# Attention and two mixture-of-experts layers in one kernel: w1 split by quarters, scatters without a wait between halves, and the first expert's weight splits of layer 2 moved

## The reference

```
cur = np.einsum('bhd,bhe->bhde', u[None] * kt, vt)
y[:, :, t] = np.einsum('bhd,bhde->bhe', rt, state + cur)
state = wt[:, :, :, None] * state + np.einsum('bhd,bhe->bhde', kt, vt)
...
h = np.maximum(x[mask] @ w1[e], 0.0)
out[mask] = gate_w[mask, None] * (h @ w2[e])
...
for k in range(2):
    mask = top2[:, k] == e
    h = np.maximum(x[mask] @ w1[e], 0.0)
    out[mask] += top2_w[mask, k, None] * (h @ w2[e])
```

## Time and profile before

| | us |
|---|---|
| median of 3 runs (lowest, highest) | 1000.42 (1000.36, 1000.91) |
| time of the profiled execution | 1001.47 |
| its span in the profile | 999.8 |
| TensorE matmul busy | 910.0 |
| VectorE busy | 540.0 |
| ScalarE busy | 228.8 |
| GpSimd busy | 350.7 |
| mean granted TensorE clock, share of full | 0.958 |

### The profile page before, as it was taken

The page is one execution under the profiler, slowest core; times in us unless marked ns, Lnnn a source line. Parts: engine busy times, 40 slices in busy tenths (PEclk is TensorE's granted clock), DMA queues, the critical chain, the costliest instruction groups (busy, mean ns, idle before and its releaser), DMA issues.

```text
span 999.8 us, 22055 instructions
## 1 busy us (share of the span) xinstructions
PE 910.0 (91%) x7285; PEld 881.0 (88%) x7286; DVE 540.0 (54%) x950; ACT 228.8 (23%) x417; POOL 350.7 (35%) x364
## 2 busy tenths in 40 slices
PE   5999999999999999681499999999999999999994
PEld 5888888899999999571499899998998999999894
DVE  8888998784333343249753444435436354543532
ACT  2232333112110121154121312213113131311210
POOL 7333334324322223103434343433534343343232
PEclk9999998999999999795599999999999999999998
DMA  6676782129111102451263444424424444422232
GB/s 246 203 233 217 267 279 78 54 60 360 49 49 40 55 32 64 123 182 47 52 211 56 106 104 115 100 52 108 110 40 102 118 102 114 106 48 42 39 55 42
DMA packets 54447, 111.46 MB, mean 111 GB/s; under 512 B 8688, under 2 KB 35568, under 8 KB 54384
## 3 DMA queue, kind: packets, MB, share of 16 engines
q1 hardware_dynamic: 34752, 71.07, 21.4%
q0 software_dynamic: 15744, 34.70, 17.2%
q10 hardware_dynamic: 3888, 4.89, 1.3%
HBM read 84.84 MB, written 25.81 MB: 111 GB/s over the span
## 4 chain that ended last, share of the span: by engine, by line
PE 85%; DVE 10%; issue 2%; DMA 2%; ACT 0%; DVEq 0%; POOL 0%; POOLq 0%
PE ps L1640 22%; PE ps L1642 22%; PE ps L1641 22%; PE ps L1550 3%; PE ps L1510 2%; PE ps L1514 2%; PE ps L1479 2%; PE ps L1456 2%; DVE weights L1089 2%; PE ps L1541 2%; PE ps L1504 1%; PE ps L1565 1%; PE ps L1577 1%; DVE grow L893 1%; PE ps L1464 1%
## 5 line engine op out<-in xcount | busy, mean ns | idle before, releaser
L1640 PE MATMUL ps<-x_hi,weights 128*128 128x256 f32 x984 | 280.1, 285 | 12.3 <-DVE x_lo L1361 12.3
L1642 PE MATMUL ps<-x_hi,weights 128*128 128x256 f32 x984 | 279.2, 284 | 0.0
L1641 PE MATMUL ps<-x_lo,weights 128*128 128x256 f32 x984 | 279.1, 284 | 0.0
L822 ACT ACTIVATE hid_hi<-ps 128x512 fp32r<-128x512 f32 x164 | 98.3, 599 | 567.3 <-PE ps L1642 567.3
L1640 PE MATMUL ps<-weights,hid_hi 128*128 (+1 forms) x616 | 214.2, 348 | 1.4 <-DVE hid_lo L1366 1.1
L1366 DVE SCALAR_TENSOR_TENSOR hid_lo<-ps,hid_hi 128x512 fp32r<-128x512 f32 x164 | 112.7, 689 | 184.4 <-ACT hid_hi L822 184.4
L1642 PE MATMUL ps<-weights,hid_lo 128*128 (+1 forms) x616 | 207.3, 337 | 0.0
L1641 PE MATMUL ps<-weights,hid_hi 128*128 (+1 forms) x616 | 207.2, 336 | 0.0
L1640 PEld LDWEIGHTS ps<-x_hi,weights 128*128 128x128 f32 x984 | 188.2, 191 | 14.4 <-DVE x_lo L1361 11.4
L1641 PEld LDWEIGHTS ps<-x_lo,weights 128*128 128x128 f32 x984 | 188.4, 191 | 0.0
L1642 PEld LDWEIGHTS ps<-x_hi,weights 128*128 128x128 f32 x984 | 188.2, 191 | 0.0
(11 more groups left out here) (279 smaller groups left out, 1076.8 us busy)
## 6 DMA issues: line engine op xcount, KB each, us to landing
stage<-in_moe_w_dram SPq DMA_DIRECT2D x18, 1536.0 KB, 7.4
kv_in<-in_kv_T_dram SPq DMA_DIRECT2D x24, 512.0 KB, 5.6
kv_in<-in_kv_T_dram SPq DMA_DIRECT2D x24, 448.0 KB, 3.5
w_in<-in_w_T_dram SPq DMA_DIRECT2D x24, 258.5 KB, 4.2
out_dram<-zeros SPq DMA_DIRECT2D x25, 192.0 KB, 8.5
x_rows<-y_tok ACTq DMA_DIRECT2D x24, 192.0 KB, 4.7
stage<-moe_rows SPq DMA_DIRECT2D x12, 384.0 KB, 5.0
stage<-in_moe_w_dram SPq DMA_DIRECT2D x2, 768.0 KB, 7.7
```

What stands on the lines that cost most here:

```text
L822: act.activation(hid_hi[:, 2 * q:2 * q + 2, :], h_ps[q], ACT.Relu).then_inc(s_hhi[l], 1)
L1640: pe.matmul(out_ps, hi, by_hi, start=first, stop=False)
L1641: pe.matmul(out_ps, hi, by_lo, start=False, stop=False)
L1642: return pe.matmul(out_ps, lo, by_hi, start=False, stop=final)
```

## The change

There are three parts. **w1 by quarters:** at a change, ScalarE copies quarter q of w1 right behind `hidden_high(s, q)` and VectorE subtracts it right behind `hidden_low(s, q)`; TensorE waits for each quarter by itself. The same holds for the first expert of layer 2. In layer 1's first expert the halves stay. The first `split_x` now stands behind the fourth `hidden_low`, and VectorE's lookups behind the first one instead of the second. **Spare rows:** the empty places of the second half of a step name another 128 rows, `out` is 128 rows longer, and the wait between a step's two scatters is gone; the scatters of a step wait for both scatters of the step before. **Start of layer 2:** GpSimd's `split_w2(0)` stands behind the third gather, two quarters of VectorE's `low_w1` ahead of the lists' code and two behind the `split_x`, and `low_w2` behind `slot_tables`.

```diff
-        spare_row = [sb("spare_row0", [P, NTX[0]]), sb("spare_row1", [P, 1])]
+        spare_row = [sb("spare_row0", [P, NTX[0]]), sb("spare_row1", [P, TS])]
...
+        def w1_quarter(tile, at, q):
+            return tile[:, at:at + WSZ].rearrange("p (c f) -> p c f", c=CC)[:, :, q * F // 4:(q + 1) * F // 4]
...
                     load_w2(l, e)
-                    sp.wait_ge(s_w1lo[l], n * 2)
+                    sp.wait_ge(s_w1lo[l], n * 4)
...
-                    for g in range(G + 1):
+                    for g in range(G + TS):
                         clear(g)
...
                 if l == 1:
-                    split_w2(0)
                     pool.wait_ge(s_table[l], 1)
...
                     if l == 1 and not (isinstance(s, int) and s == 0):
-                        pool.wait_ge(s_scatter[l][1 - u][TS - 1], j * 16 + u * 16)
+                        for t in range(TS):
+                            pool.wait_ge(s_scatter[l][1 - u][t], j * 16 + u * 16)
...
                         else:
-                            if t > 0:
-                                pool.wait_ge(s_scatter[l][u][t - 1], j * 16 + 16)
-                                pool.nop(nofuse=True)
                             pool.indirect_dma_start(out=out, out_offset=where, in_=sy[u][:, t, 0:C], in_offset=None,
...
                 if l == 0:
                     first_w2()
                 else:
+                    split_w2(0)
                     pool.wait_ge(s_table[l], 3)
...
+            def split_w1(l, n, q):
+
+                act.wait_ge(s_w1[l], loaded(l, n, 1))
+                act.activation(w1_quarter(weights, W1_HI, q), w1_quarter(w1_raw, 0, q), ACT.Copy).then_inc(s_w1hi[l], 1)
...
-                    for q in range(1, 4):
-                        hidden_high(s, q)
-                    with act.If(change > 0):
-                        act.wait_ge(s_h[l], s * 4 + 4)
-                        act.nop(nofuse=True)
-                        for a in range(2):
-                            split_w1(l, run + 1, a)
+                    for q in range(4):
+                        if q:
+                            hidden_high(s, q)
+                        with act.If(change > 0):
+                            split_w1(l, run + 1, q)
...
-                    low_w1(1, 0, 0)
-                    low_w1(1, 0, 1)
+                    for q in range(2):
+                        low_w1(1, 0, q)
                     dve.wait_ge(s_code[l], 1)
...
                     split_x(0, 0, 0)
                     split_x(0, 0, 1)
+                    for q in range(2, 4):
+                        low_w1(1, 0, q)
+                    slot_tables(1)
                     low_w2(1, 0)
-                    slot_tables(1)
                     loop_ends(1)
...
                     hidden_low(s, 0)
-                    hidden_low(s, 1)
                     if runs_from(l, s):
...
+                        for q in range(4):
+                            if q:
+                                hidden_low(s, q)
+                            if q == 3:
+                                split_x(s + 1, 1 - u, 0)
+                            with dve.If(change > 0):
+                                low_w1(l, run + 1, q)
...
                     if runs_from(l, s):
-                        with dve.If(change > 0):
-                            for a in range(2):
-                                low_w1(l, run + 1, a)
                         split_x(s + 1, 1 - u, 1)
...
                 def up(s, q, run):
 
-                    pe.wait_ge(s_w1lo[l], run * 2 + 2)
+                    pe.wait_ge(s_w1lo[l], 4 if l == 0 and isinstance(s, int) and s == 0 else run * 4 + q + 1)
                     pe.wait_ge(s_sxc[l], s * TS + TS)
```

More of the change, by code:

```diff
@@ L685, in _ @@
                     pool.wait_ge(s_mixst, 16)
-                    pool.wait_ge(s_zero, 16 * (G + 1))
+                    pool.wait_ge(s_zero, 16 * (G + TS))
                     gather(0, 0, 0)
@@ L746, in attention_step @@
                 if late(b, c) in (6, 7):
-                    split_w1(0, 0, late(b, c) - 6)
+                    first_w1(late(b, c) - 6)
                 if late(b, c) in (8, 9):
@@ L1339, in _ @@
                        .then_inc(s_table[l], 1)
-                    link(dve.tensor_scalar(idx_tmp[:, 0:NSl], empty[:, 0:NSl], spare_row[l][:, 0:1], None, ALU.mult))
+                    link(dve.tensor_tensor(idx_tmp[:, 0:NSl].rearrange("p (s t) -> p s t", t=TS),
+                                           empty[:, 0:NSl].rearrange("p (s t) -> p s t", t=TS),
+                                           spare_row[l][:, :].unsqueeze(1).to_broadcast([P, NSX[l], TS]), ALU.mult))
                     link(dve.tensor_tensor(idx_tmp[:, 0:NSl], idx_tmp[:, 0:NSl], second[:, 0:NSl], ALU.add))
@@ L1405, in slot_step @@
                         change, fresh = lookup(dve, w1_now[l], s, 1), lookup(dve, w2_now[l], s, 1)
-                    hidden_low(s, 2)
-                    split_x(s + 1, 1 - u, 0)
-                    hidden_low(s, 3)
+                        for q in range(4):
+                            if q:
[4 more added lines that the diff above has]
+                                low_w1(l, run + 1, q)
+                    else:
+                        hidden_low(s, 1)
+                        hidden_low(s, 2)
+                        split_x(s + 1, 1 - u, 0)
+                        hidden_low(s, 3)
                     if runs_from(l, s):
-                        with dve.If(change > 0):
-                            for a in range(2):
-                                low_w1(l, run + 1, a)
                         split_x(s + 1, 1 - u, 1)
```

26 lines of the change are left out of this document (15 added, 11 removed).

## The result

The changed kernel takes 986.32 us, the median of 4 runs (985.32 to 988.84), against 1000.40 for the kernel before (4 runs beside it, 1000.36 to 1000.91): a ratio of 0.9861, 95% interval 0.9843 to 0.9878. The forecast was 985.1. The profiled execution is 985.47 us with a span of 983.7; before they were 1001.47 and 999.8. Two later measurements of the same file gave ratios of 0.9880 (0.9863 to 0.9896) and 0.9894 (0.9872 to 0.9916), because the change had medians 1.5 and 1.1 us higher there (987.80 and 987.44) and the kernel before 1.4 and 3.3 us lower ones (999.0 and 997.1), with single runs from 993.8 to 1001.2: its first four lay unusually close together. The ratios differ a little from those of the medians. The gain is 10 to 14 us.

The account below looks back on a forecast made before the run. TensorE bounds the kernel (85% of the span), so only its idle or low-clock time can be gained. 7.6 + 1.55 + 4.5 - 1.1 + 2.8 = 15.35 us takes the median from 1000.42 to 985.1, range 980.5 to 991.

Parts of the forecast that it names:

- Quarter operations: Copying and subtracting w1 by quarters: 0.94 us each on VectorE, 0.8 on ScalarE.
- Short steps with a change: Four short steps of layer 2 where w1 changes: 1.9 us less TensorE idle time each, 7.6 in all.
- The next `up` starts at about 561.4: At the layer 2 change profiled at 558 us: `up` starts there in place of 563.31, 1.9 gained.
- Layer 1's change: Layer 1's one change of w1: idle 1.69 less a transposes' wait of 0.15, 1.55 us gained.
- Clock behind changes: Behind three layer 2 changes TensorE's clock no longer falls: 1.5 us each, 4.5 in all.
- Start of layer 2: Gathers 3.15 us earlier, but GpSimd holds VectorE's tables; `down` stalls 2.7, clock costs 1.5: net -1.1 us.
- four rows where the hold happened: Evidence cited, at layer 2's start, that GpSimd's subtraction holds VectorE, against the rival without such a hold.
- Scatters: End of layer 2: second scatter starts 3.24 us earlier, less 0.4 for a stretched landing, 2.8 gained.
- The start of layer 2 keeps its gain: Rival at layer 2's start: clock holds, 983.6 us; without GpSimd's hold too, 980.9; chance 0.22.
- Dear quarters: Rival: a VectorE quarter takes as long as a half, 995.1 us; chance 0.15, shared with clock losses kept.
- transfers in series: Rival at the end: both halves' accumulating transfers run in series, nothing gained there, 988 us; chance 0.08.
- TensorE's register instructions per quarter: Slower rival: 123 of them in 41 steps stop TensorE's matmul queue; at 0.15 us each 1003.6; chance 0.03.

Follow-up runs that it names:

- E6: The change, with TensorE's second register load of a step moved behind `up`; 986.24 us, ratio 0.9887 to the kernel before.
- E2: The kernel before with only the spare rows and the free second scatter; 994.43 us, ratio 0.9960.
- E3: The kernel before with only the moved split of w2 at the start of layer 2; 996.43 us, ratio 0.9973.
- E1: The kernel before with only w1's quarters and their places in the steps; 991.15 us, ratio 0.9921.
- E7: The change, with the next step's first rows split ahead of VectorE's last `hidden_low`; 988.62 us, ratio 0.9900 to the kernel before.
- E5: The change, with GpSimd waiting for the slot tables before its subtraction of the first w2; 985.55 us, ratio 0.9876 to the kernel before.
- E8: The change, with VectorE's first two `hidden_low` ahead of its lookups in layer 2's first step; 987.00 us, ratio 0.9882 to the kernel before.
- E10: The change with the edits of E5 and E6 together; 980.76 us, ratio 0.9832 to the kernel before.
- E9: The change, with all four low w1 quarters of layer 2's first expert ahead of the lists' code; 986.15 us, ratio 0.9883 to the kernel before.

## Why the prediction was right, and where it was not

**The time was right, 985.1 against 986.3 (and 987.8 and 987.4 later); the total hides errors of both signs.** The profiled execution was forecast at 986.1 and is 985.5, but 2.6 us of its 16 come from the attention stage, which the change doesn't touch. Without them the change gave 13.5 where 15.35 were summed. The gain itself, forecast at 15.3, measured 14.1 beside the first four runs and about 12 and 10.5 by the later ratios. That the median fell within 1.2 us of the forecast is in part luck.

- *Quarter operations:* 0.95 and 0.84 against 0.94 and 0.8. Right. For VectorE the line through two other widths was enough; ScalarE's was a choice within a range.
- *Short steps with a change:* forecast 1.9 each, 7.6 in all; measured 1.4 each, 5.5. The mis-sized step is the sentence "The next `up` starts at about 561.4". VectorE's side was if anything too dear: the second transposes wait 0.42 to 0.67, not 0.8. But with VectorE out of the way, TensorE's own two lookups became the last to finish. They stand in the trace of before at 560.4 and 561.1, inside the stall that was to vanish, and the prediction asked only what VectorE would be late with. E6 shows it: with the second lookup moved, 2.3 us come back.
- *Layer 1's change:* 1.55 forecast. The idle time fell by 1.43, the place moved by 1.1. In this profile the gate's wait for its rows grew from 9.79 to 11.08 and took that back. In the eleven profiles with this edit the wait is 9.70 to 11.08, 10.4 in the mean, and in the three without it (the kernel before, E2, E3) 9.35 to 10.00, 9.7 in the mean. So part of this term may never reach the gate; that the wait follows from the change isn't shown.
- *Clock behind changes:* 4.5 forecast, 4.5 in the pair of profiles. But the falls are not the same from one execution of the kernel before to the next: E2 and E3, with the same stalls, show it behind two of four. Against a typical execution of the kernel before the term is nearer to 3. E1, priced at 13.65 by the prediction's sum, measured 7.9 (6.6 to 9.2): its profiled execution is 10.2 shorter than that of before, but the median of the kernel before in that job lies 2.45 below its profiled execution. One fall less, 1.5, is part of this; the rest stays open.
- *Start of layer 2:* -1.1 forecast. Every step of the chain came as told: `mix` 0.18, the store's landing deciding the gathers, `slot_cmp` held for 3.76 (about 3.5 foreseen). The instant that `down` waits for was right to 0.1 us (12.85 behind `up` forecast, 12.76 measured). The stall was to be 2.7 with a clock loss of 1.5; it is 1.22 without one, 2.23 with one, 2.02 with one, and 2.00 and 2.14 with one in E6 and E7. It is shorter because `up` itself took longer: the prediction kept the 2.9 us after which the clock had come back in the kernel before, and in the change it took 3.3 to 5.5. Against the 3.3 to 4.4 gained ahead of `up`, the place is worth from -0.8 to +0.5 in the three profiles of the change; other kernels with the same code ahead of `up` (E5 to E8, E10) gained 1.3 to 3.4 there, so this term is known to about 2 us only. E3 and E5 show that it takes the hold and a late `hidden_low` 1 together. The prediction's "four rows where the hold happened" are two in the rows that it names, `mix` and `row_mix`.
- *Scatters:* 2.8 forecast with 0.4 for a stretched landing; 3.3 measured, the landing unstretched (5.4 behind the last issue against 5.5). E2 measured 4.0 (2.3 to 5.7) for this part alone.
- *The rivals.* "The start of layer 2 keeps its gain" is not what the change does, but it is what the code does with the edit alone (E3) or with one line moved (E5). Dear quarters and transfers in series are out by the rows above. TensorE's register instructions per quarter cost nothing that shows: an ordinary full step takes 17.5 to 17.6 from `up` to `up` before and after, without idle time, and E1 gains 0.79%. A lookup is another matter, 0.31 per load.

## What to carry to other kernels

When a stall goes, list what every engine did during it, the waiting engine's own queue first: register loads that were free in its shadow are next in line, and they can often be moved under other work. Where two engines hold each other, removing one meeting makes another, and a hold costs nothing as long as nobody is waiting (3.87 us of it in E3): look for the instruction that somebody waits for and let it pass first, rather than try to avoid the hold (one swapped pair of lines took 2.0 to 3.7 us off the stretch behind it). And take the clock's losses from several executions: a term read from one profile can be half again too large.

## What the runs showed that was not expected

- **The hold goes both ways.** In the change GpSimd's subtraction takes its usual 3.5 and VectorE's `slot_cmp` 3.76. In E5 VectorE's `low_w2` starts 0.17 ahead, runs at its usual 1.75, and GpSimd's takes 4.94. The Trainium skill (SBUF — State Buffer, who interferes with whom) calls the shared ports an exclusive lock that goes to whoever issues first. By the recorded starts, the rows of E5, of the change (GpSimd 489.72, `slot_cmp` 489.77) and of the kernel before (475.13, 475.27) agree. Those of E3 and E9 do not: `more` stands 0.32 ahead of GpSimd's subtraction in both (490.35 and 490.67; 491.06 and 491.38) and is the held one, 3.87 and 3.89. Whether GpSimd's recorded start is late or the rule is not the whole of it stays open.
- **Two numbers can be held, one not.** Beside the same GpSimd instruction, `even_i` on 128x1 int32 took 0.15 and on 128x2 int32 2.72, a TENSOR_SCALAR with one input. The same page says that a `tensor_scalar` can enter a two-port mode and then contends; that the second element is what lets it in is my reading, and no run tests it.
- **Register loads have a price on each engine.** 0.31 per load on TensorE; VectorE's three with their branches show as 1.37 of idle time between two `hid_lo` (E9), and as none in E5, where VectorE was held just ahead of them.
- **The clock comes back at different times.** Behind the idle stretch before layer 2's first `up` it was back at 2.4 GHz 2.9 us after `up` began in the kernel before, and 3.3 to 5.5 after in three profiles of the change, at half speed until then. What decides it stays open. 2.6 us more at half speed make `up` 1.3 us longer; where `down` waits for VectorE anyway, as in the change, the time goes into the stall instead.
